# Last stage's three first products by a 2x2 block scheme with seven block products, in groups of 1,024 tokens

## Chip, cores and metric

One core of a Trainium2 chip runs the kernel. The metric is the time of one execution in microseconds (us), the median of several runs. TensorE is called PE here, VectorE DVE, ScalarE ACT, GpSimd POOL and SyncE SP.

## What is computed

Three stages follow each other over 3,072 tokens of 512 features: windowed attention, a mixture of experts that sends every token to one of eight experts, and a dense stage that takes the elementwise maximum of three products and multiplies it by a fourth matrix. Only the last stage is changed:

```python
def _moe2_setup():
    n_tokens, d_model, d_ff = (3072, 512, 768)

def _moe2_ref(x, w1, w2, w3, w_out) -> np.ndarray:
    h = np.maximum(np.maximum(x @ w1, x @ w2), x @ w3)
    return (h @ w_out).astype(np.float32)
```

## The kernel before

All engines run programs written out by hand, joined by semaphores. Every engine takes its instructions strictly in order, so an instruction that waits holds up all that stands behind it on that engine.

Every float32 product is made of three: an operand is split into a high part (a copy rounded to the type F32R, made by ACT) and a low part (the operand less its high part, made by DVE), and `three` (L1068) accumulates low by high, high by low and high by high in one PSUM bank.

The last stage works on six groups of 512 tokens (`GT`, `NG`). All its weights are brought in by six transfers of 1,024 KB (`load_fin`, L378), and are split once (`split_fin` L614, `low_fin` L864), and their two parts stay in SBUF for all groups. For a group, `group` on PE (L1139) runs over six blocks `f` of 128 hidden features. For each of the three matrices it accumulates four K-blocks, by three, in one bank: 12 matmuls of 128x512. ACT copies the first bank (`f_a`, L667), DVE takes the maximum with the second and then the third (L920, L923), ACT makes the high part of the result (L669) and DVE the low part (L925). One block later `out_product` (L1126) multiplies these by the fourth matrix: 12 matmuls per block, into four banks that stay open for the whole group. The rows of the next group are transposed on PE in between (`fturn`, L1112), four transposes at each of four blocks, and split by ACT (L672) and DVE (L930). Rows come in and results leave by transfers of 1,024 KB that SP issues; the last group's results go in four transfers of 256 KB.

Between the expert stage and the last stage PE runs 26 unused matmuls (`keep_warm`, L1048) and waits for the last rows of the expert stage to land in DRAM. Then the first 512 rows are loaded in four transfers, transposed and split tile by tile (L1120 to L1124, L660, L910), before the first product.

In the expert stage SP loads 512 KB of weights at a time (`load_chunk`, L397 to L401), from DRAM rows of 4 KB for each partition. DVE opens that stage with `split_w(0, 0)`, `split_w(0, 1)` and `split_x(0)` just ahead of its loop.

Of the kernel before, what the change touches and what calls it, by code (L numbers as in the profile page):

```python
# [14 lines left out]
P = 128  # L15
# [41 lines left out]
GT = 512  # L57
TG = GT // P
NG = NT // GT
FC = NMAT * KD * P + DM  # L60
# [21 lines left out]
def build(nc, qT, kT, vW, w9, wpack, wfin, out):  # L82
# [6 lines left out]
    with ctx:  # L89
# [12 lines left out]
        with ExitStack() as landing:  # L102

            sb, _ = tensors(landing)
            fin_raw = sb("fin_raw", [P, FB2, FC])
            x_buf = sb("x_buf", [P, NTT, DM])

        with ExitStack() as early:
            sb, _ = tensors(early)  # L110
            far = [(sb(f"q_sb{i}", [P, S]), sb(f"k_sb{i}", [P, 2, KCOLS]), sb(f"v_sb{i}", [P, 2, NCH, DV]))
                   for i in (2, 3)]
        sb, _ = tensors(ctx)
# [43 lines left out]
        with ExitStack() as moe:  # L157
            sb, ps = tensors(moe)
            w_hi = [sb(f"w_hi{i}", [P, CHK], F32R) for i in range(RING)]
# [11 lines left out]
            g_in = sb("g_in", [P, TB])  # L171
# [42 lines left out]

        with ExitStack() as fin:
            sb, ps = tensors(fin)
            f_in = [sb(f"f_in{i}", [P, TG, DM]) for i in range(2)]
            f_xhi = [sb(f"f_xhi{i}", [P, KD, GT], F32R) for i in range(2)]
            f_xlo = [sb(f"f_xlo{i}", [P, KD, GT], F32R) for i in range(2)]
            f_a = sb("f_a", [P, GT])  # L220
            f_b = sb("f_b", [P, GT])
            f_h = sb("f_h", [P, GT])
            f_hhi = [sb(f"f_hhi{i}", [P, GT], F32R) for i in range(2)]
            f_hlo = [sb(f"f_hlo{i}", [P, GT], F32R) for i in range(2)]
            f_out = sb("f_out", [P, TG, DM])
            ps_m = [ps(f"ps_m{i}", [P, GT]) for i in range(NMAT)]
            ps_f = [ps(f"ps_f{i}", [P, DM]) for i in range(TG)]
            ps_fx = ps("ps_fx", [P, GT])
# [10 lines left out]
        s_wfin = [sem(f"s_wfin{i}") for i in range(FB2)]  # L239
        s_fhi = sem("s_fhi")  # L240
        s_flo = sem("s_flo")
# [62 lines left out]

        s_first = [sem(f"s_first{i}") for i in range(TG)]
        s_fin = [sem(f"s_fin{i}") for i in range(2)]
        s_ftr = sem("s_ftr")
        s_fxhi = sem("s_fxhi")
        s_fxlo = sem("s_fxlo")
        s_fm = sem("s_fm")  # L310
        s_fa = sem("s_fa")
        s_fb = sem("s_fb")
        s_fh = sem("s_fh")
# [3 lines left out]
        s_fo_a = sem("s_fo_a")  # L317
        s_fo_v = sem("s_fo_v")
        s_fst = sem("s_fst")
        s_ofree = sem("s_ofree")  # L320
# [11 lines left out]
        def fin_w(w, m, k, f):  # L332
            at = (m * KD + k) * P
            return w[:, f, at:at + P]

        def fin_wout(w, f):
            return w[:, f, NMAT * KD * P:]

        def first_turned(t):  # L340
            return (ps_m + [ps_fx])[t][:, :].rearrange("p (k c) -> p k c", k=KD)

        def first_rows(x, t):
            return x[:, :, t * P:(t + 1) * P]
# [10 lines left out]
        def _(sp):  # L355
# [22 lines left out]
            def load_fin(f):  # L378
                sp.dma_start(fin_raw[:, f, :], wfin[f]).then_inc(s_wfin[f], 16)
# [12 lines left out]
            load_fin(0)  # L392
# [22 lines left out]

            sp.wait_ge(s_landed, count + 1)
            sp.sem_inc(s_pass, 1)
            sp.wait_ge(s_whi, count * FB + LEAD)
            sp.sem_inc(s_pass, 1)
            sp.wait_ge(s_wlo, count * FB + RAW + LEAD - 1)  # L420
            sp.sem_inc(s_pass, 1)
            sp.wait_ge(s_xlo, count * 2 + 2)
            for t in range(0, TG, 2):
                sp.dma_start(f_in[0][:, t, :], x_f[0][:, t, :]).then_inc(s_first[t], 16)
            load_fin(1)
            sp.dma_start(f_in[1][:, :, :], x_f[1]).then_inc(s_fin[1], 16)
            for f in range(2, FB2):
                load_fin(f)

            def rows_of(x, n):  # L430
                if isinstance(n, int):
                    return x[n]
                return x[bass.ds(n, 1)].rearrange("a p t c -> (a p) t c")

            def rows_and_store(g, par, more):
                if more and not (isinstance(g, int) and g == 0):
                    sp.wait_ge(s_ftr, g * KD + KD)
                    sp.dma_start(f_in[1 - par][:, :, :], rows_of(x_f, g + 1)).then_inc(s_fin[1 - par], 16)
                if not more:
                    for t in range(TG):  # L440
                        sp.wait_ge((s_fo_a, s_fo_v)[t % 2], g + 2 + t // 2)
                        sp.dma_start(out_f[g][:, t, :], f_out[:, t, :]).then_inc(s_fst, 16)
                    return
                sp.wait_ge(s_fo_a, g + 2)
                sp.wait_ge(s_fo_v, g + 2)
                sp.dma_start(rows_of(out_f, g), f_out[:, :, :]).then_inc(s_fst, 16)
                sp.wait_ge(s_fst, g * 16 + 16)
                sp.sem_inc(s_ofree, 1)

            rows_and_store(0, 0, True)  # L450
            with sp.Fori(0, NG // 2 - 1) as i:
                rows_and_store(i * 2 + 1, 1, True)
                rows_and_store(i * 2 + 2, 0, True)
            rows_and_store(NG - 1, 1, False)
            sp.wait_ge(s_fst, 16 * (NG - 1 + TG))

# [128 lines left out]
        def _(act):  # L585
# [28 lines left out]
            def split_fin(f):  # L614
                act.wait_ge(s_wfin[f], 16)
                act.activation(fin_hi[:, f, :], fin_raw[:, f, :], ACT.Copy).then_inc(s_fhi, 1)

            act.wait_ge(s_xst, 16 * B)
            split_fin(0)
# [18 lines left out]
            split_x()  # L638
            with act.Fori(0, count) as i:
# [12 lines left out]
            act.sem_inc(s_ofree, 1)  # L652
# [3 lines left out]
            for t in range(1, TG, 2):  # L656
                act.dma_start(f_in[0][:, t, :], x_f[0][:, t, :]).then_inc(s_first[t], 16)
            for t in range(TG):
                act.wait_ge(s_ftr, t + 1)
                act.activation(first_rows(f_xhi[0], t), first_turned(t), ACT.Copy).then_inc(s_fxhi, 1)  # L660

            def group(g, par, more):
                for f in range(FB2):
                    if isinstance(g, int) and g == 0 and f + 1 < FB2:
                        split_fin(f + 1)
                    act.wait_ge(s_fm, (g * FB2 + f) * NMAT + 1)
                    act.activation(f_a[:, :], ps_m[0][:, :], ACT.Copy).then_inc(s_fa, 1)  # L667
                    act.wait_ge(s_fh, g * FB2 + f + 2)
                    act.activation(f_hhi[f % 2][:, :], f_h[:, :], ACT.Copy).then_inc(s_fhhi, 1)  # L669
                    if more and 1 <= f <= KD:  # L670
                        act.wait_ge(s_ftr, g * KD + KD + f)
                        act.activation(f_xhi[1 - par][:, f - 1, :], ps_fx[:, :], ACT.Copy).then_inc(s_fxhi, 1)  # L672

                if not more:
                    act.wait_ge(s_ofree, g + 1)
                    for t in range(0, TG, 2):
                        act.wait_ge(s_ff, g + t + 1)
                        act.activation(f_out[:, t, :], ps_f[t][:, :], ACT.Copy).then_inc(s_fo_a, 1)
                    return
                act.wait_ge(s_ff, g + 1)  # L680
# [13 lines left out]
        def _(dve):  # L694
# [209 lines left out]
            for s in (s_fxlo, s_fb, s_fh, s_fa, s_fo_a, s_fo_v):  # L904
                dve.sem_inc(s, 1)
# [309 lines left out]
```

## Time and profile before

| | us |
|---|---|
| median of 3 runs | 745.48 (744.73 to 746.19) |
| the profiled execution | 744.42 |
| its span, first to last instruction | 742.3 |
| PE busy | 714.5 (96%) |
| DVE busy | 322.6 (43%) |
| ACT busy | 229.6 (31%) |
| last stage, first product to last | 327.6 to 739.1 |

The profile counts an engine as busy while one of its instructions runs; matmuls overlap, so a busy time of 395 ns for one stands beside a distance of 233 ns from the start of one to the start of the next. DMA share is the mean busy share of 16 DMA engines. PEclk is the granted clock of TensorE, where 1.00 is 2.4 GHz and 0.50 is 1.2 GHz.

### The profile page before, as it was taken

What the parts mean: (1) busy time and instruction counts of PE and PEld (TensorE: products, weight loads), DVE (VectorE), ACT (ScalarE), POOL (GpSimd) and SP (SyncE); (2) the same over time, 40 slices, a digit from 0 to 9 for tenths busy, and PEclk for the clock granted to TensorE, in tenths of its full rate; (3) what the DMA queues carried; (4) which work ended last, traced back from release to release, by engine and by line L of the source; (5) the groups of instructions that cost most, each with busy time, mean ns of one, the idle gap of its engine ahead of it and who ended that gap; (6) DMA issues with size and microseconds to landing.
All of it is one profiled execution on the core that took longest, in us unless ns stands there. A gap on an engine that the chain in (4) does not pass through costs nothing.

```text
span 742.3 us, 13113 instructions
## 1 busy us (share of the span) xinstructions
PE 714.5 (96%) x5065; PEld 585.2 (79%) x5065; DVE 322.6 (43%) x565; ACT 229.6 (31%) x363; POOL 126.0 (17%) x153
## 2 busy tenths in 40 slices
PE   5999966999999999979999999999999999999998
PEld 4777644999999999968888888888888888888886
DVE  4777766666666666644432212222122222222112
ACT  4554533555555555523311111111111111111111
POOL 7211113344446445410000000000000000000000
PEclk9999986999999999999999999999999999999999
DMA  8999955666566565472003000300020020001001
GB/s 312 414 312 306 348 181 187 221 204 206 185 242 210 204 202 165 137 283 121 0 1 114 0 1 1 113 1 1 32 81 0 0 82 31 0 0 57 0 1 57
DMA packets 31114, 93.01 MB, mean 125 GB/s; under 512 B 5036, under 2 KB 5164, under 8 KB 30320
## 3 DMA queue, kind: packets, MB, share of 16 engines
q1 hardware_dynamic: 27504, 87.12, 33.3%
q0 software_dynamic: 3296, 5.00, 1.9%
q10 hardware_dynamic: 288, 0.52, 0.2%
q8 instruction: 19, 0.31, 0.2%
q14 instruction: 7, 0.06, 0.0%
HBM read 79.77 MB, written 16.79 MB: 130 GB/s over the span
## 4 chain that ended last, share of the span: by engine, by line
PE 93%; DVE 2%; DMA 2%; issue 1%; POOL 1%; SPq 0%; ACT 0%; DVEq 0%; POOLq 0%
PE ps_m L1070 14%; PE ps_m L1072 14%; PE ps_m L1071 14%; PE ps_f L1072 5%; PE ps_f L1071 5%; PE ps_f L1070 5%; PE ps_h L1070 4%; PE ps_h L1072 4%; PE ps_h L1071 4%; PE ps_y L1070 4%; PE ps_y L1071 4%; PE ps_y L1072 4%; PE ps_o L1012 3%; PE ps_s L965 3%; PE ps_xT L999 2%; PE ps_pT L977 2%
## 5 line engine op out<-in xcount | busy, mean ns | idle before, releaser
L1070 PE MATMUL ps_m<-f_xhi,fin_lo 128*128 128x512 f32 x432 | 170.6, 395 | 1.6 <-DVE f_xlo L910 1.6
L1072 PE MATMUL ps_m<-f_xhi,fin_hi 128*128 128x512 f32 x432 | 170.6, 395 | 0.0
L1071 PE MATMUL ps_m<-f_xlo,fin_hi 128*128 128x512 f32 x432 | 170.5, 395 | 0.0
L854 DVE TENSOR_TENSOR w_lo<-raw,w_hi 128x1024 fp32r<-128x1024 f32 x66 | 81.9, 1252 | 52.3 <-ACT w_hi L628 52.3
L920 DVE TENSOR_TENSOR f_b<-ps_m,f_a 128x512 f32<-128x512 f32 x36 | 24.9, 692 | 178.5 <-PE ps_m L1072 178.4
L1070 PEld LDWEIGHTS ps_m<-f_xhi,fin_lo 128*128 128x128 f32 x432 | 81.1, 188 | 21.2 <-DVE f_xlo L910 1.8
L1072 PEld LDWEIGHTS ps_m<-f_xhi,fin_hi 128*128 128x128 f32 x432 | 81.1, 188 | 19.6
L1071 PEld LDWEIGHTS ps_m<-f_xlo,fin_hi 128*128 128x128 f32 x432 | 81.1, 188 | 19.6
L628 ACT ACTIVATE w_hi<-raw 128x1024 fp32r<-128x1024 f32 x67 | 71.0, 1059 | 52.9 <-PE ps_y L1072 50.5
L669 ACT ACTIVATE f_hhi<-f_h 128x512 fp32r<-128x512 f32 x36 | 22.8, 632 | 206.7 <-DVE f_h L923 206.7
L1070 PE MATMUL ps_h<-x_hi,w_lo 128*128 128x256 f32 x256 | 72.2, 282 | 0.3 <-DVE x_lo L861 0.3
L1072 PE MATMUL ps_h<-x_hi,w_hi 128*128 128x256 f32 x256 | 72.4, 283 | 0.0
L1071 PE MATMUL ps_h<-x_lo,w_hi 128*128 128x256 f32 x256 | 72.4, 283 | 0.0
L1070 PE MATMUL ps_f<-fin_hi,f_hlo 128*128 128x512 f32 x144 | 58.3, 405 | 0.0
L923 DVE TENSOR_TENSOR f_h<-ps_m,f_b 128x512 f32<-128x512 f32 x36 | 24.9, 692 | 75.9 <-PE ps_m L1072 75.9
L1072 PE MATMUL ps_f<-fin_hi,f_hhi 128*128 128x512 f32 x144 | 56.8, 394 | 0.0
L1071 PE MATMUL ps_f<-fin_lo,f_hhi 128*128 128x512 f32 x144 | 56.7, 394 | 0.0
L667 ACT ACTIVATE f_a<-ps_m 128x512 f32<-128x512 f32 x36 | 21.5, 597 | 110.7 <-PE ps_m L1072 110.7
L1070 PEld LDWEIGHTS ps_h<-x_hi,w_lo 128*128 128x128 f32 x256 | 48.9, 191 | 3.2 <-DVE x_lo L861 0.8
L1070 PE MATMUL ps_y<-w_hi,h_lo 128*128 128x512 f32 x128 | 51.3, 401 | 0.0
L1071 PEld LDWEIGHTS ps_h<-x_lo,w_hi 128*128 128x128 f32 x256 | 48.9, 191 | 2.2
L1071 PE MATMUL ps_y<-w_lo,h_hi 128*128 128x512 f32 x128 | 50.4, 394 | 0.0
(147 smaller groups left out, 949.4 us busy)
## 6 DMA issues: line engine op xcount, KB each, us to landing
raw<-wpack SPq DMA_DIRECT2D x67, 512.0 KB, 4.0
v_sb<-vW SPq DMA_DIRECT2D x32, 390.0 KB, 4.9
k_sb<-kT SPq DMA_DIRECT2D x32, 250.0 KB, 4.8
q_sb<-qT SPq DMA_DIRECT2D x16, 384.0 KB, 5.9
x_dram<-x_buf SPq DMA_DIRECT2D x4, 1536.0 KB, 9.4
fin_raw<-wfin SPq DMA_DIRECT2D x6, 1024.0 KB, 11.8
f_in<-x_dram SPq DMA_DIRECT2D x5, 1024.0 KB, 5.5
out<-f_out SPq DMA_DIRECT2D x5, 1024.0 KB, 4.2
```

What stands on the lines that cost most here:

```text
L628: act.activation(w_hi[c % RING][:, :], raw[:, c % RAW, :], ACT.Copy).then_inc(s_whi, 1)
L667: act.activation(f_a[:, :], ps_m[0][:, :], ACT.Copy).then_inc(s_fa, 1)
L669: act.activation(f_hhi[f % 2][:, :], f_h[:, :], ACT.Copy).then_inc(s_fhhi, 1)
L854: dve.tensor_tensor(w_lo[c % RING][:, :], raw[:, c % RAW, :], w_hi[c % RING][:, :].bitcast(F32), ALU.subtract).then_inc(s_wlo, 1)
L920: dve.tensor_tensor(f_b[:, :], ps_m[1][:, :], f_a[:, :], ALU.max).then_inc(s_fb, 1)
L923: dve.tensor_tensor(f_h[:, :], ps_m[2][:, :], f_b[:, :], ALU.max).then_inc(s_fh, 1)
L965: last = pe.matmul(ps_s[g % 2][CHUNK * r:CHUNK * (r + 1), t, :, :], q_sb[j][:, c * CHUNK:(c + 1) * CHUNK], k_sb[j][:, :, c * BLOCK:c * BLO ...
L977: last = pe.transpose(ps_pT[:, t * P:(t + 1) * P], prob[g % 2][:, t, :, :].rearrange("p w h -> p (w h)"), ident[:, :])
L1012: last = pe.matmul(ps_o[g % 2][CHUNK * r:CHUNK * (r + 1), t, :, :], probT[:, t, CHUNK * r:CHUNK * (r + 1)], v_sb[j][:, :, c, :], start=Tru ...
L1070: pe.matmul(out_, a_lo, b_hi, start=first, stop=False)
L1071: pe.matmul(out_, a_hi, b_lo, start=False, stop=False)
L1072: return pe.matmul(out_, a_hi, b_hi, start=False, stop=end)
```

## The change

The last stage now takes three groups of 1,024 tokens. The tokens are halved, the 512 features are halved, and the hidden features are taken in pairs of 128-blocks. So `x` has quarters A11, A12 (first 512 tokens), A21, A22 (last 512), and a weight has quarters B11, B12, B21, B22 of 256x128 each. One *unit* is one matrix and one pair of blocks: nine units for a group (`UNITS`), 27 in all, numbered `n`. Instead of eight block products a unit has seven, of 6 matmuls of 128x512 each. In PE's order and with their banks they are P1 = A11·B11 (`ps_c`), P2 = A12·B21 (`ps_a`), P3 = S2·T2 (onto P1), P4 = S1·T1 (`ps_b`), P5 = S3·T3 (onto P3), P6 = S4·B22 (onto P4), P7 = A22·T4 (onto P5). S1 to S4 are sums of quarters of `x`, made once a group. T1 to T4 are sums of quarters of the weight and are made by DVE for every unit (`unit_sums`); then ACT makes the high parts of seven blocks (`unit_high`) and DVE their low parts (`unit_low`).

Weights no longer stay in SBUF: `load_unit` brings 512 KB for every unit, 27 times, into one of two buffers `u_f`. The tensors named in the `bits` block stand at the same addresses as those that `fin` opens with, in the same order, so `u_f` is `u_lo`, and `h_f` is `f_hlo`. The partial results are copied from the bank by ACT before the next product is accumulated onto it (`copy_p1`, `copy_u2`, `copy_p5`, `copy_u3`), and DVE adds the copies and takes the maxima (`quarter_11` to `quarter_21`). The output products run at the end of each group, one tile of 128 tokens after the other (`rows_out`, 18 matmuls each), with the transposes of the next group between them. Eight tiles must be transposed before the first product of the stage instead of four. In the expert stage's prelude DVE runs `unit_sums(0)` and ACT `unit_high(0)`.

The diff, cut to its core:

```diff
-GT = 512
+GT = 1024
+HT = GT // 2
+UNITS = FB2 // 2 * NMAT
+KH = KD // 2
+OUTS = 4
...
+        with ExitStack() as bits:
+            sb, _ = tensors(bits)
+            sb("c_hi_f", [P, 7, KH, HT])
+            sb("c_lo_f", [P, 7, KH, HT])
+            h_hi_f = sb("h_hi_f", [P, FB2, GT])
+            h_f = sb("h_f", [P, FB2, GT])
+            u_f = [sb(f"u_f{i}", [P, 8, KH * P]) for i in range(2)]
+            o_f = sb("o_f", [P, FB2, DM])
         with ExitStack() as fin:
...
+            c_hi = sb("c_hi", [P, 7, KH, HT], F32R)
+            c_lo = sb("c_lo", [P, 7, KH, HT], F32R)
+            f_hhi = sb("f_hhi", [P, FB2, GT], F32R)
+            f_hlo = sb("f_hlo", [P, FB2, GT], F32R)
+            u_lo = [sb(f"u_lo{i}", [P, 8, KH * P], F32R) for i in range(2)]
+            o_lo = sb("o_lo", [P, FB2, DM], F32R)
+            u_hi = [sb(f"u_hi{i}", [P, 7, KH * P], F32R) for i in range(2)]
...
         def _(sp):
...
+            def load_unit(n):
+                sp.dma_start(u_f[n % 2][:, 0:4, :], wunit[n % UNITS].rearrange("p (b c) -> p b c", b=4))\
+                    .then_inc(s_uload[n % 2], 16)
...
+            for g in range(NG):
+                for u in range(UNITS):
+                    n = g * UNITS + u
+                    if n + 2 < NG * UNITS:
+                        sp.wait_ge(s_prod, n * 7 + 7)
+                        load_unit(n + 2)
+                for t in range(TG):
+                    if t == TG // 2 and g + 2 < NG:
+                        load_rows(g + 2)
+                    store(g, t)
...
         def _(act):
...
+            def unit_high(n):
+                act.wait_ge(s_usum, n * 4 + 4)
+                act.activation(u_hi[n % 2][:, :, :], u_f[n % 2][:, 1:8, :], ACT.Copy).then_inc(s_uhi, 1)
...
+            def copy_u2(n, s):
+                if n % UNITS >= 2:
+                    act.wait_ge(s_m12, n - 1)
+                act.wait_ge(s_prod, n * 7 + 3)
+                act_copy(f_u2[s][:, :], ps_c[s][:, :]).then_inc(s_u2, 1)
...
+            def unit(g, u):
+                n, s = g * UNITS + u, u % 2
+                closed = u >= 1 and (u - 1) % NMAT == NMAT - 1
+                copy_p1(n, s)
+                if n + 1 < NG * UNITS:
+                    unit_high(n + 1)
+                copy_u2(n, s)
+                if closed:
+                    h_high_11(n - 1)
+                copy_p5(n, s)
+                if closed:
+                    h_high_22(n - 1)
+                copy_u3(n, s)
+                if closed:
+                    h_high_12(n - 1)
+                    h_high_21(n - 1)
...
         def _(dve):
...
+            def unit_sums(n):
+                w = u_f[n % 2]
+                dve.wait_ge(s_uload[n % 2], n // 2 * 16 + 16)
+                dve.tensor_tensor(w[:, T1, :], w[:, B12, :], w[:, B11, :], ALU.subtract).then_inc(s_usum, 1)
+                dve.tensor_tensor(w[:, T3, :], w[:, B22, :], w[:, B12, :], ALU.subtract).then_inc(s_usum, 1)
+                dve.wait_ge(s_usum, n * 4 + 1)
+                dve.tensor_tensor(w[:, T2, :], w[:, B22, :], w[:, T1, :], ALU.subtract).then_inc(s_usum, 1)
+                dve.wait_ge(s_usum, n * 4 + 3)
+                dve.tensor_tensor(w[:, T4, :], w[:, B21, :], w[:, T2, :], ALU.subtract).then_inc(s_usum, 1)
...
+            def unit_low(n):
+                dve.wait_ge(s_uhi, n + 1)
+                dve.tensor_tensor(u_lo[n % 2][:, 1:8, :], u_f[n % 2][:, 1:8, :], u_hi[n % 2][:, :, :].bitcast(F32),
+                                  ALU.subtract).then_inc(s_ulo, 1)
...
             split_w(0, 0)
+            unit_sums(0)
+            split_x(0)
             split_w(0, 1)
-            split_x(0)
...
+            def unit(g, u):
+                n = g * UNITS + u
+                closed = u >= 1 and (u - 1) % NMAT == NMAT - 1
+                if u >= 1:
+                    quarter_21(n - 1)
+                if 0 < n < NG * UNITS - 1:
+                    unit_sums(n + 1)
+                if n > 0:
+                    quarter_11(n)
+                if n + 1 < NG * UNITS:
+                    unit_low(n + 1)
...
+                if closed:
+                    h_low(n - 1, 0)
+                    h_low(n - 1, 1)
+                quarter_22(n)
+                quarter_12(n)
+                if closed:
+                    h_low(n - 1, 2)
+                    h_low(n - 1, 3)
+                if g == 0 and 1 <= u <= FB2:
+                    out_low(u - 1)
...
         def _(pe):
...
+            def product(bank, c, b, n, first):
+                w = n % 2
+                for k in range(KH):
+                    last = three(bank[:, :], u_hi[w][:, b - 1, k * P:(k + 1) * P], u_lo[w][:, b, k * P:(k + 1) * P],
+                                 c_hi[:, c, k, :], c_lo[:, c, k, :], first and k == 0, k == KH - 1, not first)
+                last.then_inc(s_prod, 1)
...
+            def unit(g, u):
+                n, s = g * UNITS + u, u % 2
+                pe.wait_ge(s_ulo, n + 1)
...
+                product(ps_c[s], A11, B11, n, True)
...
+                product(ps_a[s], A12, B21, n, True)
...
+                pe.wait_ge(s_p1, n + 1)
+                product(ps_c[s], S2, T2, n, False)
...
+                product(ps_b[s], S1, T1, n, True)
...
+                pe.wait_ge(s_u2, n + 1)
+                product(ps_c[s], S3, T3, n, False)
...
+                pe.wait_ge(s_p5, n + 1)
+                product(ps_b[s], S4, B22, n, False)
...
+                pe.wait_ge(s_u3, n + 1)
+                product(ps_c[s], A22, T4, n, False)
```

## Rows read from the trace of the kernel before

**Rows 1.** The page's part 4: the chain that ended last, by engine.

```profile
PE 93%; DVE 2%; DMA 2%; issue 1%; POOL 1%; SPq 0%; ACT 0%; DVEq 0%; POOLq 0%
```

**Rows 2.** Stretches: start:end length, busy us (count) by engine, PEclk, DMA share, GB/s.

```profile
327.60:738.90 411.30, 411.28 (x1808) 332.27 (x1808) 105.31 (x144) 69.48 (x109) 0.00 (x0) 1.00 0.09 36
```

**Rows 3.** Timeline of PE, steady part: start, duration, engine, line, operation.

```profile
430.23 0.39 PE L1070 MATMUL ps_m<-f_xhi,fin_lo 128*128 128x512 f32 x1
430.46 0.40 PE L1071 MATMUL ps_m<-f_xlo,fin_hi 128*128 128x512 f32 x1
430.69 0.39 PE L1072 MATMUL ps_m<-f_xhi,fin_hi 128*128 128x512 f32 x1
...
431.12 0.60 ACT L667 ACTIVATE f_a<-ps_m 128x512 f32<-128x512 f32 x1 [4.16 <-PE ps_m L1072]
```

**Rows 4.** The page's groups: busy us, mean ns of one, idle before.

```profile
L1070 PE MATMUL ps_m<-f_xhi,fin_lo 128*128 128x512 f32 x432 | 170.6, 395 | 1.6 <-DVE f_xlo L910 1.6
L1070 PE MATMUL ps_f<-fin_hi,f_hlo 128*128 128x512 f32 x144 | 58.3, 405 | 0.0
L920 DVE TENSOR_TENSOR f_b<-ps_m,f_a 128x512 f32<-128x512 f32 x36 | 24.9, 692 | 178.5 <-PE ps_m L1072 178.4
```

**Rows 5.** Groups by shape, for durations at other widths.

```profile
L881 DVE SCALAR_TENSOR_TENSOR h_lo<-ps_h,h_hi 128x256 fp32r<-128x256 f32 x64 | 26.7, 417 | 8.7 <-ACT h_hi L642 8.7
L866 DVE TENSOR_TENSOR fin_lo<-fin_raw,fin_hi 128x2048 fp32r<-128x2048 f32 x6 | 13.8, 2292 | 10.1 <-ACT fin_hi L616 6.5 <-POOLq L581 3.7
L628 ACT ACTIVATE w_hi<-raw 128x1024 fp32r<-128x1024 f32 x67 | 71.0, 1059 | 52.9 <-PE ps_y L1072 50.5 <-DMA raw<-wpack 2.4
L616 ACT ACTIVATE fin_hi<-fin_raw 128x2048 fp32r<-128x2048 f32 x6 | 11.4, 1907 | 7.3 <-DMA fin_raw<-wfin 7.3
```

**Rows 6.** Line L400, loads of 512 KB: first of 280 to 305 us, then all 67.

```profile
DMA to landing us min/median/max: 3.2/3.3/4.5
...
DMA to landing us min/median/max: 3.2/4.0/5.7
```

**Rows 7.** DMA issues: KB each, median us from issue to landing.

```profile
f_in<-x_dram SPq DMA_DIRECT2D x5, 1024.0 KB, 5.5
out<-f_out SPq DMA_DIRECT2D x4, 256.0 KB, 2.1
```

**Rows 8.** Timeline of DVE, then SP: a store that waits for DVE.

```profile
396.71 1.29 DVE L941 COPY f_out<-ps_f 128x512 f32<-128x512 f32 x2 [3.44 <-PE ps_f L1072]
...
398.09 0.40 SPq L446 DMA_DIRECT2D out<-f_out  x1
```

**Rows 9.** Timeline at the start of the last stage.

```profile
320.32 0.81 SPq L424 DMA_DIRECT2D f_in<-x_dram  x2
...
323.70 1.07 PE L1123 MATMUL ps_m<-ident,f_in 128*128 128x128 f32 x8 [2.49 <-DMA f_in<-x_dram]
...
325.00 1.97 DVE L910 TENSOR_TENSOR f_xlo<-ps_m,f_xhi 128x512 fp32r<-128x512 f32 x3 [2.85 <-ACT f_xhi L660]
...
325.44 0.60 PE L1123 MATMUL ps_fx<-ident,f_in 128*128 128x128 f32 x4
...
327.62 0.50 PE L1070 MATMUL ps_m<-f_xhi,fin_lo 128*128 128x512 f32 x1 [1.57 <-DVE f_xlo L910]
```

**Rows 10.** Timeline at the expert stage's start: DVE's splits and PE's second weights.

```profile
122.46 2.29 DVE L854 TENSOR_TENSOR w_lo<-raw,w_hi 128x1024 fp32r<-128x1024 f32 x2
...
126.79 1.29 DVE L861 TENSOR_TENSOR x_lo<-ps_x,x_hi 128x512 fp32r<-128x512 f32 x2 [2.04 <-ACT x_hi L632]
...
128.94 0.28 PE L1072 MATMUL ps_h<-x_hi,w_hi 128*128 128x256 f32 x1
```

**Rows 11.** Stretches, as Rows 2: where PE is idle, and the granted clock.

```profile
312.00:327.60 15.60, 11.37 (x59) 9.04 (x57) 8.47 (x11) 4.41 (x8) 2.02 (x2) 1.00 0.44 162
...
5.00:12.00 7.00, 4.18 (x75) 3.10 (x75) 2.51 (x7) 1.77 (x4) 6.99 (x6) 1.00 0.95 334
12.00:20.00 8.00, 7.70 (x141) 5.96 (x141) 4.87 (x15) 2.86 (x6) 3.04 (x4) 0.79 1.01 410
```

More of the change, by code:

```diff
@@ L218, in build @@
[L218 to L226, printed above, removed]
@@ L316, in build @@
         s_ff = sem("s_ff")
[L317 to L320, printed above, removed]
+        s_out = sem("s_out")
+        s_ost = [sem(f"s_ost{i}") for i in range(OUTS)]
         x_b = x_dram.rearrange("(b t p) c -> b p t c", b=B, p=P)
@@ L425, in _ @@
[L425 to L448, printed above, removed]
@@ L458, in _ @@
+            for i in range(OUTS):
+                sp.wait_ge(s_ost[i], 16 * NG * TG // OUTS)
         @block.gpsimd
@@ L638, in _ @@
             split_x()
+            unit_high(0)
             with act.Fori(0, count) as i:
@@ L656, in _ @@
             for t in range(1, TG, 2):
[L657 to L680, printed above, removed]
-                act.wait_ge(s_ofree, g + 1)
-                for t in range(TG // 2):
-                    last = act.activation(f_out[:, t, :], ps_f[t][:, :], ACT.Copy)
-                last.then_inc(s_fo_a, 1)
@@ L944, in _, with low @@
-            group(0, 0, True)
-            with dve.Fori(0, NG // 2 - 1) as i:
-                group(i * 2 + 1, 1, True)
-                group(i * 2 + 2, 0, True)
-            group(NG - 1, 1, False)
+            dve.sem_inc(s_pass, 1)
+            dve.wait_ge(s_whi, count * FB + LEAD)
+            unit_low(0)
+            unit_sums(1)
+            def low(c, k, x, highs):
+                dve.wait_ge(s_chi, highs)
+                dve.tensor_tensor(c_lo[:, c, k, :], x, c_hi[:, c, k, :].bitcast(F32), ALU.subtract)\
+                    .then_inc(s_clo, 1)
@@ L951, in _ @@
+            first_sums()
+            for g in range(NG):
+                for u in range(UNITS):
+                    unit(g, u)
+                n = g * UNITS + UNITS - 1
+                quarter_21(n)
+                for which in range(4):
+                    h_low(n, which)
+                if g + 1 < NG:
+                    turned(g + 1, 0)
+                    turned(g + 1, 1)
         @block.tensor
@@ new lines, in turn_quarter, with turn_rows @@
+            def turn_quarter(bank, i, k):
+                for t in range(TH):
+                    last = pe.transpose(bank[:, t * P:(t + 1) * P], f_in[:, i * TH + t, k * P:(k + 1) * P], ident[:, :])
+                return last
+            def turn_rows(g, k):
+                if k == 0:
+                    pe.wait_ge(s_fin, 16 * g)
+                    pe.wait_ge(s_m11, g * UNITS)
+                    pe.wait_ge(s_m12, g * UNITS - 1)
+                    pe.wait_ge(s_m21, g * UNITS - 1)
+                else:
+                    pe.wait_ge(s_clo, g * 14 + 7)
+                turn_quarter(turn_a11, 0, k)
+                turn_quarter(turn_a21, 1, k)
+                turn_quarter(turn_a22, 1, KH + k)
+                turn_quarter(turn_a12, 0, KH + k).then_inc(s_ftr, 1)
@@ new lines, in rows_out @@
+            def rows_out(t, f0, f1):
+                for f in range(f0, f1):
+                    last = three(out_bank(t)[:, :], f_hhi[:, f, t * P:(t + 1) * P], f_hlo[:, f, t * P:(t + 1) * P],
+                                 o_hi[:, f, :], o_lo[:, f, :], f == 0, f == FB2 - 1)
+                if f1 == FB2:
+                    last.then_inc(s_ff, 1)
+            first_rows()
+            for g in range(NG):
+                for u in range(UNITS):
+                    unit(g, u)
+                if g + 1 < NG:
+                    turn_rows(g + 1, 0)
+                if g == 0:
+                    pe.wait_ge(s_olo, FB2)
+                else:
+                    pe.wait_ge(s_out, g * TG)
+                pe.wait_ge(s_fhlo, g * 12 + 8)
+                rows_out(0, 0, FB2 - 2)
+                rows_out(1, 0, FB2 - 2)
+                pe.wait_ge(s_fhlo, g * 12 + 12)
+                rows_out(0, FB2 - 2, FB2)
+                rows_out(1, FB2 - 2, FB2)
+                pe.wait_ge(s_m12, g * UNITS + UNITS)
+                rows_out(2, 0, FB2)
+                if g + 1 < NG:
+                    turn_rows(g + 1, 1)
+                pe.wait_ge(s_m21, g * UNITS + UNITS)
+                rows_out(3, 0, FB2)
+                pe.wait_ge(s_out, g * TG + 3)
+                rows_out(4, 0, FB2)
+                pe.wait_ge(s_out, g * TG + 4)
+                rows_out(5, 0, FB2)
+                pe.wait_ge(s_out, g * TG + 1)
+                rows_out(6, 0, FB2)
+                pe.wait_ge(s_out, g * TG + 2)
+                rows_out(7, 0, FB2)
```

489 lines of the change are left out of this document (329 added, 160 removed).

## The prediction, made before the changed kernel was run

> **What bounds the kernel now.** I read the chain of waits first: PE carries 93% of it [rows 1]. Then the stretch from the last stage's first product to its last: in 411.3 us PE is busy for 411.28, DVE for 105 and ACT for 69, at a granted clock of 1.00 [rows 2]. So in this stage nothing but PE sets the time, and DVE and ACT have room. The timeline gives the price of one matmul of 128x512: they start 0.233 us apart (430.23, 430.46, 430.69), though each is drawn 0.39 long [rows 3]. The stage has 3x432 of them into `ps_m` and 3x144 into `ps_f` [rows 4], 1,728 in all, or 402.6 us; 80 transposes fill the rest. The timeline also gives the hand-off: the last matmul of a bank starts at 430.69 and ACT reads the bank at 431.12, so a result is ready 0.2 us after the next product could have started [rows 3].
>
> **Removed.** A unit has 7 products of 6 matmuls, and there are 27 units: 1,134 matmuls in place of 1,296. The 162 that go are all on PE's path: 162 x 0.233 = 37.8 us. The output products stay 432, and the transposes stay 96 with those ahead of the first product. A product lasts 1.40 us and a unit 9.8 us if PE never waits.
>
> **DVE's and ACT's added work.** I price DVE by width: 0.42 us for 256, 0.69 for 512, 2.29 for 2,048, so 2.0 for 1,792 [rows 4, 5]. Neighbours that don't depend on each other start 0.64 apart at 512 wide (three in 1.97) [rows 9]. Three units (29.4 us of PE) ask of DVE 12 weight sums (5.0), 3 low parts of 1,792 (6.1), 17 sums and maxima of 512 (11.7) and 4 low parts of h (2.8): 25.6 us. That fits, as a mean. ACT has 1.06 us for 1,024 and 1.91 for 2,048 [rows 5], so 1.7 for `unit_high`, and 0.6 for each copy of 512 [rows 3]: some 15.4 us per three units. Neither engine becomes the bound by its load. The order within a unit decides.
>
> **The added wait: one weight load in every unit.** `u_lo` lies on top of `u_f`, so the load of unit n+1 can't start before unit n-1 has made its last product. SP waits for just that. Behind the load stands a chain, and PE's P5 of unit n stands at its end. The queues make it so: on ACT `copy_u2(n)` is behind `unit_high(n+1)`, which waits for DVE's four sums, which wait for the load; and PE's P5 waits for `copy_u2(n)`, with P6 and P7 behind it. Count from the end of unit n-1's last matmul:
> - SP's answer: 0.1 us (DVE ends at 398.00, SP issues at 398.09) [rows 8];
> - issue to landing of 512 KB: 3.3 us, the median late in the expert stage; over all such loads it is 4.0, the shortest 3.2 [rows 6]. Between 280 and 305 us there is the least other traffic, and in the last stage the DMA engines have next to nothing else (share 0.09) [rows 2], so I take 3.3;
> - DVE's start 0.1, four sums of 256 at 0.42, where only the first pair can overlap: 1.6;
> - `unit_high(n+1)` 1.7, `copy_u2(n)` 0.6, hand-offs 0.05.
>
> That is 7.45 us. Without it P5 would start four products (5.6 us) after P1, and P1 starts 0.16 before the point I count from: 5.44. PE stands for 2.0 us in the unit. What follows doesn't add: `unit_low(n+1)` runs beside P5 and P6 and is done before the next P1; copies of P4 and P5 have 1.4 us each; and DVE's remaining pieces, also the four low parts of h where a pair closes, end before the next load has landed. The unit takes 11.8 us instead of 9.8. Nothing catches up, since the next load is issued only when this unit is over.
>
> How many units pay: the load is early only for those behind a group boundary (n = 9, 18), where some 34 us of output products lie between, and n = 26 has no successor. Unit 0 and unit 1 are counted below. That leaves 2 to 8, 10 to 17 and 19 to 25: 22 units, 44.0 us. If the landing is 4.0, the stall is 2.7 and the sum 59; if it is 3.2 and the sums take 1.5, it is 1.8 and 40.
>
> **The start of the stage.** Before, four tiles of rows are in at about 325.4, and the tile-by-tile splits let PE start at 327.62 [rows 9]. Now PE's queue has eight tiles ahead of P1. From 1,024 KB in 5.5 us [rows 7] against 512 KB in 3.3 [rows 6] another 1 MB costs 4.2 us: the last tile lands at about 329.5, and P1 starts at 330.0: +2.4. In unit 0 the sums of `x` are made under way. After the transposes ACT has two copies, `unit_high(1)` and two high parts (4.1 us), and DVE six sums and then two low parts at 0.64: P3 can start at 336.0 instead of 332.8. Before P6 and P7 the same queues cost 1.3 and 0.5 more. Unit 0 is stretched by 5.0, `unit_low(1)` (2.0 us, the last of that queue) holds unit 1 by 0.5, and unit 1's own stall is then 1.4. Together 9.3 us; between 5 (if the pieces overlap better) and 12 (if the second megabyte comes at the rate of loads under traffic).
>
> **Edits priced at nothing.** In the expert stage's prelude `unit_sums(0)` moves `split_x(0)` not at all (DVE idles 2.04 us before it), but `split_w(0, 1)` now ends at about 129.3, where PE wants these weights at 128.9 [rows 10]: 0.4 us. At the group boundaries the transposes and the first output tiles (7 us of PE) cover the low parts of the last h blocks (done 4.4 us after the unit), and 34 us of output products cover the 14 low parts of the next rows. The stores of 256 KB go out under the next tile; the last one ends like the one before, 2.1 us after its issue [rows 7].
>
> **Sum.** 742.3 - 37.8 + 9.3 + 0.4 + 44.0 = 758.2 us of span. Around its span the profiled execution has 2.1 us (744.42), and the median is 1.1 above that execution, so 758.2 + 3.2 = 761.4. With the bounds of landing and start: 742.3 - 37.4 + 5 + 40 + 3.2 = 753, and 742.3 - 37.4 + 12 + 59 + 3.2 = 779.
>
> **Rivals.**
> - *The load lands sooner, and the kernel is faster.* The place is `unit_sums`' wait. The saving of 37.8 less 9.7 pays for a stall of 1.28 us in 22 units, so it decides at a landing of 2.6 us; below that the change wins. With the 2.1 us of the 256 KB stores [rows 7] the stall is 0.8 and the time 742.3 - 28.1 + 17.6 + 3.2 = 735; without any stall it would be 717. For it: the DMA engines have nothing else to do. Against it: none of 67 loads of this size took under 3.2 [rows 6]. Chance 0.12, a sixth of it so near the break-even that no difference shows.
> - *The clock falls.* PE now idles 2 us of each 12. At the start of the kernel an idle PE was followed by a stretch with the granted clock at 0.79 over 8 us: 1.7 us lost [rows 11]. Once a unit, that is 37 us more: 799. Against it: between 312 and 327.6 PE stood for 4.2 of 15.6 us, once for 2.49 in a piece [rows 9], and the clock stayed at 1.00 [rows 11]. Chance 0.05.
> - *The load is slower than the rows of 4 KB.* If it is broken into its four blocks of 1 KB for each partition, or the loads meet rows and stores, it costs 4.5 like the slowest late one [rows 6]: stall 3.2, 742.3 - 28.1 + 70.4 + 3.2 = 788. Against it: both sides of the transfer are contiguous for each partition. Chance 0.08.
>
> On the clock rival the Trainium skill speaks against the change: "TensorE: Matmul & The Clock Gate", section "A second HAM failure mode: psum-queue depth-cycling", describes a kernel in which short idle times between groups of matmuls made the clock swing between its two levels and cost throughput. By that rule the time would be the 799 of this rival; the stretch of 312 to 327.6 us, with 1.00 through two such idle times, does not agree [rows 11].
>
> **Chances and range.** The forecast has 0.75, rivals 0.12, 0.05 and 0.08. A measurement of this kernel tells about 0.2% from no change. Faster by more than that: 0.10; within: 0.02; slower: 0.88. The range is 749 to 779: the forecast's bounds, a little wider below for a landing between 2.9 and 3.2; rivals' times stay out of it.
>
> **What would show it.** In the profile of the changed kernel: 1,134 + 432 matmuls 0.233 apart; DVE's T1 waiting for the weight load in 23 units, some 2.5 us after `quarter_21`; an issue-to-landing time of about 3.3 for 512 KB; ACT's `unit_high` and then `copy_u2` directly behind; PE's idle time in front of the first matmul of P5, about 2 us in 22 units, released by ACT; a unit's period of 11.8 us and of 9.8 at n = 9 and 18; no idle PE in the output products; the first product at 330 us. The forecast is wrong if the load's landing is under 2.6 us, if PE waits elsewhere (P1, for `unit_low`), or if the clock leaves 1.00.

## The result, and the profile after

| | before | changed |
|---|---|---|
| median of 4, us | 745.84 (744.73 to 746.98) | 754.62 (752.88 to 757.08) |
| ratio | | 1.012, 95% interval 1.0086 to 1.0155 |
| profiled execution, its span | 742.3 | 755.3 |

The change makes the kernel 8.8 us slower; 761.4 was forecast. The profiled execution of the changed kernel is its slowest (757.08), so 13.0 us lie between the two traces and 8.8 between the medians.

The page's part 1 and two of its groups: busy time, share of the span and count; then busy us, mean ns of one, and the idle time ahead with what ended it.

```profile
PE 683.5 (90%) x4903; PEld 559.0 (74%) x4903; DVE 473.5 (63%) x811; ACT 329.8 (44%) x509; POOL 125.2 (17%) x153
...
L1332 PE MATMUL ps_c<-c_hi,u_lo 128*128 128x512 f32 x216 | 88.5, 410 | 41.2 <-ACT f_u L607 38.8
...
L636 ACT ACTIVATE u_hi<-u_f 128x1792 fp32r<-128x1792 f32 x27 | 45.9, 1698 | 65.4 <-DVE u_f L1006 65.4
```

PE has 162 matmuls less and is busy 31 us less, but it stands idle where it never did [rows 2]: 38.8 us ahead of `ps_c`'s products, released by ACT's copy `f_u`. ACT itself stood for DVE's weight sums. The view of waits gives the whole chain, with us in total, times, and the longest:

```profile
ACT u_hi L636 <- DVE u_f L1006: 65.4, 23, 3.6
...
DVE u_f L1000 <- DMA u_f<-wunit: 50.4, 23, 4.0
...
PE ps_c L1332 <- ACT f_u L607: 38.8, 23, 2.4
```

All three happen 23 times: in units 1 to 8, 10 to 17 and 19 to 25, the ones named in the forecast. One of them, unit 3, in the timelines of PE, SP, DVE and ACT:

```profile
369.59 0.39 PE L1334 MATMUL ps_c<-c_hi,u_hi 128*128 128x512 f32 x1
369.82 0.39 PE L1332 MATMUL ps_c<-c_hi,u_lo 128*128 128x512 f32 x1
...
370.01 0.33 SPq L410 DMA_DIRECT2D u_f<-wunit  x1
...
373.07 0.43 DVE L1000 TENSOR_TENSOR u_f<-u_f 128x256 f32<-128x256 f32 x1 [1.13 <-DMA u_f<-wunit]
...
374.20 0.43 DVE L1006 TENSOR_TENSOR u_f<-u_f 128x256 f32<-128x256 f32 x1
...
374.66 1.70 ACT L636 ACTIVATE u_hi<-u_f 128x1792 fp32r<-128x1792 f32 x1 [2.63 <-DVE u_f L1006]
376.27 0.58 ACT L607 ACTIVATE f_u<-ps_c 128x512 f32<-128x512 f32 x1
...
375.03 0.39 PE L1334 MATMUL ps_b<-c_hi,u_hi 128*128 128x512 f32 x1
376.90 0.50 PE L1332 MATMUL ps_c<-c_hi,u_lo 128*128 128x512 f32 x1 [1.48 <-ACT f_u L607]
377.24 0.40 PE L1333 MATMUL ps_c<-c_lo,u_hi 128*128 128x512 f32 x1
```

For all 27 loads of `u_f` the page has a median of 3.3 us from issue to landing; this one took 3.0. Unit 2's last matmul ends at 369.98 and SP issues at 370.01. The load is usable at 373.07. The sums are made by 374.63, the high parts by 376.36, and the copy by 376.85. PE has been through with P4 since 375.4 and starts P5 at 376.90. From the end of the last unit to P5: 6.9 us here; over the 22 units it is 6.9 to 7.9, with a median of 7.15. A wait also costs at its end: the matmul behind the first comes 0.34 us later and not 0.23.

The start of the stage on PE, as in [rows 9]: the first product, and unit 0's and unit 1's waits:

```profile
332.04 0.78 PE L1332 MATMUL ps_c<-c_hi,u_lo 128*128 128x512 f32 x1
...
338.06 0.50 PE L1332 MATMUL ps_c<-c_hi,u_lo 128*128 128x512 f32 x1 [2.17 <-DVE c_lo L1057]
343.65 0.50 PE L1332 MATMUL ps_b<-c_hi,u_lo 128*128 128x512 f32 x1 [1.18 <-DVE c_lo L1057]
347.08 0.51 PE L1332 MATMUL ps_c<-c_hi,u_lo 128*128 128x512 f32 x1 [0.28 <-DVE u_lo L1010]
353.83 0.50 PE L1332 MATMUL ps_c<-c_hi,u_lo 128*128 128x512 f32 x1 [0.98 <-ACT f_u L607]
```

### The profile page after: what moved, and what is told of

The parts are those of the page before. It is cut to its first block, busy times and chain, and to the rows that moved or that the text cites. A ratio compares the mean times of both kernels' runs of the same rounds, so it can differ in the third digit from the quotient of the medians.

```text
span 755.3 us, 13174 instructions
## 1 busy us (share of the span) xinstructions
PE 683.5 (90%) x4903; PEld 559.0 (74%) x4903; DVE 473.5 (63%) x811; ACT 329.8 (44%) x509; POOL 125.2 (17%) x153
## 4 chain that ended last, share of the span: by engine, by line
PE 47%; DMA 4%; issue 4%; ACT 3%; DVE 2%; POOL 0%; SPq 0%; ACTq 0%; DVEq 0%; POOLq 0%
PE ps_c L1332 8%; PE ps_c L1334 7%; PE ps_c L1333 7%; PE ps_b L1332 4%; PE ps_b L1333 4%; PE ps_b L1334 4%; PE ps_f L1332 2%; PE ps_f L1333 2%; PE ps_f L1334 2%; DMA u_f<-wunit 2%; ACT f_u L607 2%; PE ps_a L1333 1%; PE ps_a L1332 1%; PE ps_a L1334 1%; DMA x_in<-x_dram,idx_g 1%
## 5 line engine op out<-in xcount | busy, mean ns | idle before, releaser
L1332 PE MATMUL ps_c<-c_hi,u_lo 128*128 128x512 f32 x216 | 88.5, 410 | 41.2 <-ACT f_u L607 38.8
L1334 PE MATMUL ps_c<-c_hi,u_hi 128*128 128x512 f32 x216 | 85.9, 398 | 0.0
L1333 PE MATMUL ps_c<-c_lo,u_hi 128*128 128x512 f32 x216 | 85.7, 397 | 0.0
L1332 PEld LDWEIGHTS ps_c<-c_hi,u_lo 128*128 128x128 f32 x216 | 41.2, 191 | 59.9 <-ACT f_u L607 48.5
L636 ACT ACTIVATE u_hi<-u_f 128x1792 fp32r<-128x1792 f32 x27 | 45.9, 1698 | 65.4 <-DVE u_f L1006 65.4
L1010 DVE TENSOR_TENSOR u_lo<-u_f,u_hi 128x1792 fp32r<-128x1792 f32 x27 | 54.7, 2025 | 18.6 <-ACT u_hi L636 14.4
L1334 PE MATMUL ps_y<-w_hi,h_hi 128*128 128x512 f32 x128 | 50.0, 390 | 0.0
L1334 PEld LDWEIGHTS ps_h<-x_hi,w_hi 128*128 128x128 f32 x256 | 49.1, 192 | 0.0
L1333 PEld LDWEIGHTS ps_c<-c_lo,u_hi 128*128 128x128 f32 x216 | 41.4, 192 | 7.8
L1332 PE MATMUL ps_b<-c_hi,u_lo 128*128 128x512 f32 x108 | 43.9, 407 | 1.2 <-DVE c_lo L1057 1.2
```

What stands on the lines that cost most here:

```text
L636: act.activation(u_hi[n % 2][:, :, :], u_f[n % 2][:, 1:8, :], ACT.Copy).then_inc(s_uhi, 1)
L1010: dve.tensor_tensor(u_lo[n % 2][:, 1:8, :], u_f[n % 2][:, 1:8, :], u_hi[n % 2][:, :, :].bitcast(F32), ALU.subtract).then_inc(s_ulo, 1)
L1332: pe.matmul(out_, a_lo, b_hi, start=first, stop=False, skip_group_check=goes_on)
L1333: pe.matmul(out_, a_hi, b_lo, start=False, stop=False, skip_group_check=goes_on)
L1334: return pe.matmul(out_, a_hi, b_hi, start=False, stop=end, skip_group_check=goes_on)
```

## The experiments

Theory A is the one forecast: a unit's weight load can start only when the unit before the last is over, and its chain holds P5. Against it stand theory B (the added work on VectorE and ScalarE holds PE wherever the load is) and theory C (the lower clock is the larger part). Two more, D and F, came up with a number that the forecast's sum did not have.

### The load one unit earlier

```diff
-OUTS = 4
+OUTS = 2
...
-            u_f = [sb(f"u_f{i}", [P, 8, KH * P]) for i in range(2)]
+            u_f = [sb(f"u_f{i}", [P, 8, KH * P]) for i in range(3)]
...
-                    if n + 2 < NG * UNITS:
+                    if n + 3 < NG * UNITS:
                         sp.wait_ge(s_prod, n * 7 + 7)
-                        load_unit(n + 2)
+                        load_unit(n + 3)
```

> A third buffer for the weight blocks (u_f, u_lo indexed by n % 3, results buffered twice instead of four times to make room), so that the load of unit n+1 can be issued when unit n-2 is over, a whole unit earlier. Theory A, the load's chain sets the stall before P5: the 23 stalls of 1.7 us (39.8 us with unit 1's) vanish, and the median falls from 754.6 to about 715, or 710 if the clock falls of the stage go with the idle time. Theory B, the order and load of VectorE and ScalarE cost it whatever the load does: a stall of 1 to 1.7 us stays in each unit, 735 to 755. Theory C, the lower clock is the larger part: the clock falls stay and 740 or more.

Measured: 707.75 us (707.60 to 708.19), ratio to the kernel before 0.949 (0.9474 to 0.9505). PE between 345 and 700 us (start:end length, busy us and count by engine, PEclk, DMA share, GB/s), and all that was left of the wait for the copy:

```profile
345.00:700.00 355.00, 353.70 (x1585) 291.45 (x1584) 240.92 (x366) 161.20 (x235) 0.00 (x0) 1.00 0.17 58
...
PE ps_c L1333 <- ACT f_u L608: 1.0, 4, 0.3
```

The copies, sums and splits are all still there (DVE is busy 241 of 355 us), and PE waits four times for 0.25 us. So their amount isn't what costs the changed kernel; the place of the load in time is. 46.9 us are won, more than the 38.8 us of the 23 waits: the slower restart behind each wait and the clock falls of the stage go as well (PEclk 1.00). Theory B and C fall.

### ScalarE's order

```diff
                 copy_p1(n, s)
-                if n + 1 < NG * UNITS:
-                    unit_high(n + 1)
                 copy_u2(n, s)
+                copy_p5(n, s)
+                if n + 1 < NG * UNITS:
+                    unit_high(n + 1)
                 if closed:
                     h_high_11(n - 1)
-                copy_p5(n, s)
```

> The load stays as late as it is; only ScalarE's order in a unit changes: copy_u2(n) and copy_p5(n) go ahead of unit_high(n+1). Theory A says that the load is late but that PE only stands because copy_u2 is queued behind the high part that waits for it: with the copies ahead, P7 and the next unit's P1 become the first to feel the load, by 0.2 to 0.5 us a unit. About 754.6 - 22 x 1.3 = 726, or 721 if the clock falls go. Theory B (VectorE's load): 745 or more. Theory that the load itself is the cost, wherever the copies stand: 755.

Measured: 725.66 us (724.29 to 726.57). The load is issued as late as before, and 29 of 47 us are won by an order alone. PE stood because a copy that was ready to be made was queued behind a high part that was not. What is left over e1_three, 18 us, sits at P7: `copy_u3` is now behind `unit_high`. ACT's and PE's timelines, and PE's largest wait in the stage:

```profile
395.08 1.70 ACT L636 ACTIVATE u_hi<-u_f 128x1792 fp32r<-128x1792 f32 x1
396.67 0.59 ACT L607 ACTIVATE f_u<-ps_c 128x512 f32<-128x512 f32 x1
...
396.82 0.39 PE L1334 MATMUL ps_b<-c_hi,u_hi 128*128 128x512 f32 x1
397.31 0.50 PE L1332 MATMUL ps_c<-c_hi,u_lo 128*128 128x512 f32 x1
...
PE ps_c L1332 <- ACT f_u L607: 6.8, 6, 1.1
```

P7 comes 0.49 after the last matmul of P6 and not 0.23. In the six units that follow a closed pair (3, 6, 12, 15, 21, 24) two high parts of h stand in that queue as well, and PE waits 1.1 us. The expectation put this rest down to the load, and that is wrong: e8_start below has this order with the load early, and it has the same six waits and nearly the same time (724.10). The 18 us are the price of the order, not of the load.

### The load made longer

```diff
             def load_unit(n):
+                sp.dma_start(u_f[n % 2][:, 4:8, :], wunit[n % UNITS].rearrange("p (b c) -> p b c", b=4))\
+                    .then_inc(s_uload[n % 2], 16)
                 sp.dma_start(u_f[n % 2][:, 0:4, :], wunit[n % UNITS].rearrange("p (b c) -> p b c", b=4))\
                     .then_inc(s_uload[n % 2], 16)
```

> Each unit's weight transfer is followed by a second one of the same 512 KB into the half of the buffer that VectorE writes later, and VectorE waits for both. Rows of before say 2.0 us more for another 512 KB. Theory A: landing, and with it the stall, grows by 2.0 us in 23 units: 754.6 + 46 = 800, with a stall of 3.7 us before P5. If the load had room to hide, the time stays at 755. If idle time of PE lets the clock fall, there are more stretches at the lower level than in the changed kernel and the time passes 805.

Measured: 825.38 us (821.83 to 826.29), + 70.8. The waits of this run, and a stretch of the stage beside the same one of the changed kernel (first e3_double, then the changed kernel):

```profile
DVE u_f L1002 <- DMA u_f<-wunit: 87.1, 23, 5.1
...
PE ps_c L1334 <- ACT f_u L609: 70.1, 23, 3.8
```

```profile
345.00:740.00 395.00, 330.97 (x1310) 264.13 (x1309) 216.90 (x325) 139.00 (x204) 0.00 (x0) 0.89 0.22 78
```

```profile
345.00:740.00 395.00, 355.93 (x1544) 287.02 (x1543) 242.42 (x366) 156.98 (x233) 0.00 (x0) 0.98 0.15 52
```

The wait for the load grows by 1.6 us a unit (50.4 to 87.1, over 23) and PE's by 1.4 (38.8 to 70.1): what is added to the landing comes out ahead of P5. It is less than the 2.0 expected. Between the two traces lie 64.7 us of span: PE's waits are 31 of them, and the matmuls behind the waits take some 34 more, because PEclk is 0.89 here and 0.98 there. (The medians lie 70.8 apart; the other executions of e3_double have mean clocks of 0.921 to 0.927, the profiled one 0.931.) In this trace 21 of the 23 units with a wait, of 3.0 us in the mean, hold a stretch at the lower level; in the changed kernel, with 1.7 us, it is four of 23, and in e1_three none past unit 0.

### An eighth product, with the load early and with the load late

```diff
                     pe.wait_ge(s_m21, n - 1)
+                extra(ps_c[s], A11, B11, n)
                 product(ps_c[s], A11, B11, n, True)
```

> e1_three with an eighth product: PE computes A11 B11 twice in every unit (the first is overwritten). It prices the product that the scheme saves, with the load out of the way. Theory A: PE is the bound again, so e1_three + 27 x 1.40 = + 37.8 us. If VectorE or ScalarE were the bound of e1_three, part of this would be hidden and it would be + 10 to 30.

Measured: 739.25 us (738.15 to 739.84), + 31.5 over e1_three, which lies between the two expectations. 27 products at the 1.36 us that one takes in this kernel are 36.7. Two things that e1_three has and e4_eight has not make up for the rest. In unit 0 there is a stretch at the lower clock and a wait for S2 of 2.95 us against 1.78, so this unit takes 16.4 us there and 15.1 here, 2.7 less than it would with the full product added. And the four units that wait before P5 there (10.1 us) grow to 10.9 here and not by 1.36, which is another 2.2. That leaves 31.8. Past the start of unit 1 PE waits for nothing in e4_eight's products: the product is worth what it takes, as long as PE is the bound.

The same edit in the changed kernel, where the load is late:

> The changed kernel with its late load, and an eighth product in every unit (A11 B11 computed twice, ahead of P1; the first is overwritten). Theory A: the chain of the load starts at the end of the last unit and ends 7.4 us later whatever PE does, so a product of 1.36 us ahead of P1 only eats into the wait of 1.97 us: 22 units get nothing longer, five units without a wait get 1.36 each, + 7 us, less what fewer clock falls give back (up to 5): 756 to 762. So the product that the scheme saves would be worth nothing here. Theory that PE's work sets the time and the wait merely adds to it: 754.6 + 27 x 1.36 = 791.

Measured: 756.10 us (755.10 to 756.44), + 1.5 over the changed kernel; the ratio to the kernel before is 1.012 for both. The waits, in total, times and longest; a stretch; and one P5:

```profile
DVE u_f L1000 <- DMA u_f<-wunit: 50.0, 23, 3.9
...
345.00:740.00 395.00, 385.53 (x1704) 312.59 (x1703) 241.79 (x366) 157.73 (x233) 0.00 (x0) 1.00 0.16 52
...
400.42 0.50 PE L1332 MATMUL ps_c<-c_hi,u_lo 128*128 128x512 f32 x1 [0.42 <-ACT f_u L607]
```

The wait for the load is the same 50 us, and the extra 1.36 us of each unit has gone into PE's wait, 1.7 us before and 0.4 now. From the end of a unit to P5 it is 7.18 us in the median, against 7.15 in the changed kernel. The five units without such a wait pay 1.36 each (6.8), and the clock falls of the changed kernel (some 6 us in its trace) are absent: PE is through this stage at a clock of 1.00. So the eighth product, whose removal is the whole point of the scheme, costs next to nothing in the kernel as changed: the saving was spent in the wait before it could reach the end.

### Where 0.233 and 0.227 us come from

A run of products in the kernel before, in PE's timeline, and one in the changed kernel; in both the second line is 24 and 17 matmuls behind the first:

```profile
429.99 0.40 PE L1072 MATMUL ps_m<-f_xhi,fin_hi 128*128 128x512 f32 x1
...
435.59 0.40 PE L1072 MATMUL ps_m<-f_xhi,fin_hi 128*128 128x512 f32 x1
```

```profile
371.18 0.39 PE L1332 MATMUL ps_a<-c_hi,u_lo 128*128 128x512 f32 x1
...
375.03 0.39 PE L1334 MATMUL ps_b<-c_hi,u_hi 128*128 128x512 f32 x1
```

```diff
+        sb("pad", [P, 8])
```

> e1_three with 32 bytes of unused SBUF ahead of everything, so that the operands of the last stage start on multiples of 64 bytes, as in the kernel before, and not 32 past one. In the traces a 128x512 matmul starts 0.233 us after the last in the kernel before and 0.227 in the changed one, which my sum did not have. Theory D, the place of the operands modulo 64 bytes sets it: 1,566 x 0.006 = + 9 us, 717. Theory E, it is something else in the last stage's form: 707.8, no change.

> The kernel before with 32 bytes of unused SBUF ahead of its tensors, so that its operands start 32 bytes past a multiple of 64. Theory D: 1,728 matmuls start 0.227 us apart in place of 0.233, 745.9 - 10.4 = 735.5. Theory E: 745.9, no change.

Measured: 706.61 us (705.82 to 707.39) and 747.15 us (745.02 to 748.67; ratio 1.0004, 0.9988 to 1.0019). Neither moved as theory D wants. Theory F: the place of the weights against the streamed rows. In the kernel before `fin_lo` and `fin_hi` start 128 bytes past a multiple of 1,024 and the rows and h on one; in the changed kernel both kinds have the same remainder.

```diff
+        sb("pad", [P, 224])
...
         fin_lo = sb("fin_lo", [P, FB2, FC], F32R)
         fin_hi = sb("fin_hi", [P, FB2, FC], F32R)
+        sb("pad2", [P, 32])
```

> The kernel before with 896 bytes unused ahead of the last stage's weights and 128 behind them, so that weights and rows both start on multiples of 1,024 bytes; in the kernel before the weights start 128 bytes past one, while in the changed kernel all operands stand at the same place modulo 1,024. Theory F, the place of the weights relative to the streamed rows gives the 0.233 us in place of 0.227: 746 - 10 = 736. Theory E, something else of the stage's form: 746.

Measured: 737.72 us (734.45 to 738.34), ratio 0.9886 (0.9869 to 0.9903). And the other way round, in e1_three, 128 bytes between the rows' tensors and the weights':

```diff
             f_hlo = sb("f_hlo", [P, FB2, GT], F32R)
+            sb("pad", [P, 32])
```

The same 128 bytes go ahead of `u_f`, which lies under `u_lo`.

> e1_three with 128 unused bytes between the two halves of the last stage's operands: the weights' blocks (u, o) now start 128 bytes off the place of the rows (c, h) modulo 1,024. The other side of b2_offset. Theory F: 1,566 matmuls start 0.233 us apart again, + 9.2 us: 717. Theory E, that b2_offset gained by something else: 707.8, no change.

Measured: 715.08 us (714.54 to 716.16), + 7.3 over e1_three. PE's timelines of b2_offset, then of e10_offset; the second line is 17 and 24 matmuls behind the first:

```profile
429.63 0.39 PE L1074 MATMUL ps_m<-f_xhi,fin_lo 128*128 128x512 f32 x1
...
433.48 0.39 PE L1076 MATMUL ps_m<-f_xhi,fin_hi 128*128 128x512 f32 x1
```

```profile
470.32 0.39 PE L1335 MATMUL ps_b<-c_hi,u_lo 128*128 128x512 f32 x1
...
475.92 0.39 PE L1335 MATMUL ps_c<-c_hi,u_lo 128*128 128x512 f32 x1
```

3.85 / 17 = 0.226 in the kernel before, once its operands are in step, and 5.60 / 24 = 0.233 in e1_three, once they are not. Theory F holds in both directions. Why 128 bytes do that, and which remainders are good, these runs don't tell.

### The start of the stage

```diff
-                unit_high(1)
...
                 copy_u2(0, 0)
+                unit_high(1)
                 copy_p5(0, 0)
...
-                for k in range(KH):
-                    dve.tensor_tensor(first_s3[:, k, :], first_a11[k][:, :], first_s3[:, k, :], ALU.subtract)\
-                        .then_inc(s_csum, 1)
                 for k in range(KH):
                     low(S2, k, first_s2[:, k, :], 4 + k + 1)
+                for k in range(KH):
+                    dve.tensor_tensor(first_s3[:, k, :], first_a11[k][:, :], first_s3[:, k, :], ALU.subtract)\
+                        .then_inc(s_csum, 1)
```

> The three buffers of e1_three, ScalarE's order of e2_order, and the order at the start of the stage: VectorE makes the low parts of S2 before the sums S3, and ScalarE makes unit_high(1) behind copy_u2(0) and not ahead of the high parts of S2. Theory A: the small waits of e1_three before P5 (4 of 0.25) vanish, about 1 us, and P3 of unit 0 starts 1.2 us sooner; 707.8 - 2 = 706. If VectorE's load were the bound of e1_three, the start's gain would be lost later and the time would stay at 707.8 or rise.

Measured: 724.10 us (723.63 to 725.50), a miss: 16 us slower than e1_three. The waits of its trace name the copies (the view as for e2_order):

```profile
PE ps_c L1333 <- ACT f_u L608: 6.8, 6, 1.1
```

The run holds three edits, so the order of the copies was taken out again:

> e8_start with ScalarE's order in a unit back as in the changed kernel: the three buffers and the new order at the start of the stage alone. If my order of the copies was what cost e8_start its 16 us (copy_u3 behind the 1.7 us of unit_high, felt by P7 in each unit), this takes 707.8 - 1.5 = 706. If the start's order was to blame, it takes 720 or more.

Measured: 708.25 us (706.53 to 711.16), no change from e1_three. So the order of the copies that helps when the load is late costs 16 us when it is early: with the sums ready in time, `unit_high` ahead of `copy_u2` fits into ACT's idle time, and behind `copy_p5` it holds up `copy_u3`. The start's new order wins nothing that can be measured. In the profiled run of e9_three_start P3 waited 2.06 us instead of e1_three's 2.95, but matmuls 0.43 us apart, at the lower clock, ran from 339.7 to 344.6 in unit 0.

## Why the prediction was right, and its sizes

The direction, the mechanism, its place and its count were right. The closeness of the total owes something to luck, as errors of both signs met in it. Point by point:

- **The stall, 2.0 us in 22 units.** From P5 of unit 1 (353.83) to P5 of unit 6 (411.73) lie five units in 57.9 us, 11.58 each; 42 matmuls at 0.227 are 9.53. That leaves 2.05, and in the third group (636.81 to 705.63, six units) 1.94. The terms in unit 3, one of the shortest: SP 0.03, the landing with its hand-off 3.06 (3.4 forecast), the sums 1.56 (1.6), `unit_high` and copy 2.19 (2.3, as ACT starts one 0.1 before the last has ended). In the median of the 22 units the chain is 7.15, 0.3 shorter than forecast. P5 could have started 0.2 sooner and the restart after the wait costs 0.11, which makes up for it. e1_three, e3_double and e6_late_eight show that this chain, and nothing on PE, sets the unit.
- **The start, 9.3 us.** The first rows are issued 1.9 us later than in the kernel before (322.23 against 320.32 [rows 9]), and P1 starts 4.4 later: 2.5 for the four extra tiles (2.4 forecast, from 4.2 us for another 1 MB; the rows named, 5.5 and 3.3, give 4.4). Unit 0 is stretched by 5.1 (5.0), unit 1 held by 0.45 (0.5) and stretched by 1.3 up to its P5 (1.4). A stretch at the lower clock is among it, in the transposes and first products.
- **The product, 0.233 us.** This is the mis-sized term. The rows gave the price of a matmul in the old layout [rows 3], and the sum took it for all 1,566 that stay. They cost 0.227: 1,566 x 0.0062 = 9.7 us less. b2_offset and e10_offset show that it is the layout, a by-product of the change and no part of the scheme. That error did not show in the total, as the clock (+ 6.1) and the expert stage (+ 1.5 over the forecast) took most of it back: the spans are 755.3 and 758.2. The larger part of the distance from 754.6 to 761.4 is that the median was put 1.1 us above the profiled execution, as in the kernel before, and lies 2.5 below it.
- **The clock, a rival at 0.05.** It came true in part, and with it one of the forecast's own signs of being wrong, that the clock leaves 1.00: PEclk is 0.98 over the stage. In the profiled execution four units (6, 10, 11, 13) take 12.9 to 13.3 us from P5 to P5 instead of 11.5, each with a stretch at the lower level, 6.1 us in all and not the 37 of the rival. In e3_double, with 3.0 us of wait in a unit, 21 units have one. The mean clocks of the other executions are 0.980 to 0.982 against this one's 0.975, so they have less of it. The rule cited from the Trainium skill, "TensorE: Matmul & The Clock Gate", section "A second HAM failure mode: psum-queue depth-cycling", holds in kind (idle times between groups of matmuls do pull the clock down, with 0.89 in e3_double), and not at the size that a fall in every unit would have given the changed kernel.
- **A sooner load, rival at 0.12.** The shortest landing was 3.0 us, not 2.6. **A slower load, 0.08:** the median was 3.3, as the late rows of 4 KB had it [rows 6].
- **Edits at nothing.** Group boundaries cost PE nothing. The expert stage ended 1.9 us later in this execution: some 1.4 us lie ahead of its second tile (148.78 against 147.42 on the transposes), where the second weights' split was late and the clock low at the same time; 0.4 was forecast.

The sum for the two profiled spans: 742.3 - 37.7 (162 matmuls) - 9.7 (pace) + 44.0 (22 stalls, at the 2.0 that the two groups above give) + 9.3 (start, without the later issue) + 6.1 (clock in four units) + 1.9 (expert stage) = 756.2, against 755.3.

## A version that beats both

e1_three takes 707.75 us, 5.1% under the kernel before, with the same work as the changed kernel. Of that the layout's part is some 8 us by b2_offset (which puts the kernel before at 737.7) and 7 by e10_offset; the scheme with its load in time gives the other 30.

## What to carry to other kernels

When work is taken off the bound engine, look at what now has to happen between two of its steps, and add up the chain from the event that lets a transfer start to the instruction that needs it; if the chain is longer than the bound engine's work beside it, the saving is spent there, and a buffer more or an order on another engine is worth more than the saved work. A buffer shared under two names hides such a dependence: ask of each load which reader frees its place. A price read from a trace belongs to the layout it was read in.

## What the runs showed of the hardware

- Two operands of a 128x512 matmul in F32R whose places differ by 128 bytes modulo 1,024 make matmuls start 0.233 us apart, in step 0.227: 2.6%, from an unused 128 bytes (b2_offset, e10_offset). Moving all operands together by 32 bytes does nothing (e7_pad, b1_pad).
- With waits of 0.4 us in a unit (e6_late_eight) the granted clock stays at 1.00. With 1.7 us (the changed kernel) 4 of 23 units of the profiled execution have a stretch at the lower level; with 3.0 us (e3_double) 21 of 23 have one and the mean is 0.89, and from the changed kernel to e3_double the slower matmuls add some 34 us, more than the 31 of added idle time.
- A second 512 KB transfer issued right behind the first makes the pair usable 1.6 us later (e3_double), not the 2.2 that the difference of 5.5 and 3.3 in [rows 6, 7] gives or the 2.0 that was expected.
